# Stage A in seven Strassen products over pairs of token blocks, with the second block's output products moved into the next attention

## The reference, cut to what matters

```
# attention: B=4, H=8, S=768, D=64; chunks of 32 queries see 8 memory keys
# and their own chunk with 16 keys to the left and 8 to the right
for c in range(S // 32):
    scores = scale * q_c @ k_full.T            # 32 x (8 + 16 + 32 + 8) = 32 x 64 keys
    a = softmax(scores)
    out[:, :, c_start:c_end] = a @ v_full
x = out.transpose(0, 2, 1, 3).reshape(3072, 512)

# stage A: d_model 512, d_ff 1536
x = (sigmoid(x @ w_gate) * (x @ w_val)) @ w_out

# stage B: d_model 512, d_ff 2048; P and Q are polynomials in h with given coefficients
h = x @ w_in
g = P(h) / (Q(h) + 1e-6)
return g @ w_out2                              # 3072 x 512, float32
```

## Time and profile before

| | before |
| --- | --- |
| median of three runs | 1231.11 us |
| profiled execution, first to last instruction | 1228.0 us |
| TensorE matmul busy | 1201.9 us (98%) |
| VectorE busy | 733.7 us (60%) |
| ScalarE busy | 644.8 us (53%) |
| GpSimd busy | 127.5 us (10%) |
| DMA moved | 69.45 MB |
| instructions | 21612 |

### The profile page before, as it was taken

The page is one execution under the profiler, slowest core; times in us unless marked ns, Lnnn a source line. Parts: engine busy times, 40 slices in busy tenths (PEclk is TensorE's granted clock), DMA queues, the critical chain, the costliest instruction groups (busy, mean ns, idle before and its releaser), DMA issues.

```text
span 1228.0 us, 21612 instructions
## 1 busy us (share of the span) xinstructions
PE 1201.9 (98%) x8648; PEld 1001.7 (82%) x8648; DVE 733.7 (60%) x1007; ACT 644.8 (53%) x1000; POOL 127.5 (10%) x102
## 2 busy tenths in 40 slices
PE   7999999999999999999999999999999999999998
PEld 6999988878887887888888888788888888888886
DVE  4653322232223223222344599999999999999997
ACT  4654433233223332322333677777777777777775
POOL 0000000000000000000000022222222222222221
PEclk9999999999999999999999999999999999999999
DMA  5751211211211212110322300100200100100000
GB/s 190 242 182 51 99 62 44 72 51 44 87 44 39 84 44 79 45 44 1 120 95 86 112 1 1 51 18 0 68 0 0 68 0 0 68 0 0 35 1 35
DMA packets 30600, 69.45 MB, mean 57 GB/s; under 512 B 3392, under 2 KB 3392, under 8 KB 30528
## 3 DMA queue, kind: packets, MB, share of 16 engines
q1 hardware_dynamic: 30528, 68.37, 16.4%
HBM read 55.77 MB, written 12.58 MB: 56 GB/s over the span
## 4 chain that ended last, share of the span: by engine, by line
PE 51%; DVE 26%; ACT 15%; issue 3%; DMA 3%; SPq 0%; DVEq 0%; POOL 0%; ACTq 0%
DVE unit L586 12%; PE ps_h L629 11%; PE ps_h L630 10%; PE ps_h L634 10%; DVE unit L582 6%; DVE unit L579 5%; ACT unit L429 5%; PE ps_y L736 5%; PE ps_y L737 5%; PE ps_y L740 5%; ACT unit L427 4%; ACT hid L434 3%; DMA wraw<-wa_l 2%; PE ps_h L682 1%; PE ps_h L658 1%
## 5 line engine op out<-in xcount | busy, mean ns | idle before, releaser
L629 PE MATMUL ps_h<-x_split,weights 128*128 128x512 f32 (+1 forms) x1056 | 392.1, 377 | 6.3 <-issue 2.4
L630 PE MATMUL ps_h<-x_split,weights 128*128 128x512 f32 (+1 forms) x1056 | 386.0, 371 | 0.0
L634 PE MATMUL ps_h<-x_split,weights 128*128 128x512 f32 (+1 forms) x1056 | 262.7, 371 | 0.1
L302 POOL TENSOR_TENSOR unit<-unit 128x512 f32<-128x512 f32 x96 | 126.8, 1321 | 1087.2 <-ACT unit L417 1087.2
L629 PEld LDWEIGHTS ps_h<-x_split,weights 128*128 128x128 f32 x1056 | 199.4, 189 | 44.5 <-issue 7.4
L522 DVE TENSOR_TENSOR gated<-ps_h,gated 128x512 f32<-128x512 f32 (+1 forms) x84 | 51.7, 615 | 303.6 <-PE ps_h L634 296.8
L630 PEld LDWEIGHTS ps_h<-x_split,weights 128*128 128x128 f32 x1056 | 199.8, 189 | 32.4
L634 PEld LDWEIGHTS ps_h<-x_split,weights 128*128 128x128 f32 x1056 | 189.1, 189 | 34.6 <-DVE x_split L477 0.6
L586 DVE SCALAR_TENSOR_TENSOR unit<-unit,coefs 128x512 f32<-128x512 f32 x96 | 165.8, 1727 | 3.4
L361 ACT ACTIVATE hid<-gated 128x512 fp32r<-128x512 f32 (+1 forms) x84 | 47.9, 571 | 197.6 <-DVE gated L522 197.6
L355 ACT ACTIVATE gated<-ps_h 128x512 f32<-128x512 f32 (+1 forms) x84 | 45.0, 535 | 166.3 <-PE ps_h L634 166.2
(11 more groups left out here) (84 smaller groups left out, 1482.3 us busy)
## 6 DMA issues: line engine op xcount, KB each, us to landing
unit<-v_l SPq DMA_DIRECT2D x24, 520.0 KB, 5.1
unit<-k_l SPq DMA_DIRECT2D x24, 512.0 KB, 4.3
wraw<-wa_l SPq DMA_DIRECT2D x36, 256.0 KB, 3.4
wraw<-wb_l SPq DMA_DIRECT2D x32, 256.0 KB, 2.7
unit<-q_l SPq DMA_DIRECT2D x24, 256.0 KB, 2.9
y_dram<-stage SPq DMA_DIRECT2D x24, 256.0 KB, 2.3
x_stage<-y_dram SPq DMA_DIRECT2D x6, 1024.0 KB, 5.7
out<-stage SPq DMA_DIRECT2D x24, 256.0 KB, 2.2
```

The lines of the kernel that those rows point to most:

```text
L302: nc.gpsimd.tensor_tensor(quad[s], quad[s], habs[s], ALU.mult).then_inc(q2_done, 1)
L629: nc.tensor.matmul(dst, lhs(c, 0), rhs_hi(c), start=(c == 0), stop=False)
L630: nc.tensor.matmul(dst, lhs(c, 1), rhs_hi(c), start=False, stop=False)
L634: last = nc.tensor.matmul(dst, lhs(c, 0), rhs_lo(c), start=False, stop=(c == KT - 1))
```

## The change

Stage A now takes two token blocks (1024 tokens, a "super-block" `s`, three in all) and two hidden tiles at a time. The 2 x 2 grid of (token block, hidden tile), with the contraction halved as well, is one Strassen-Winograd product with seven products in place of eight: a `chain` of seven products of six matmuls each, one chain for the gate and one for the value. The four results are put together from partial sums that share PSUM banks: ScalarE takes a snapshot of a bank between two products, and VectorE adds it to another bank. The sums of weights that the method needs are made by GpSimd, the sums of x by VectorE. The weights of stage A no longer stay in SBUF: gate and value weights are loaded, summed and split for every chain (36 chains), and the output weights for every output piece (72 pieces of 256 KB) through rings of two and three buffers.

The output products of the first token block of a pair run between the chains. Those of the second block run between the steps of the next eight attention units, which are taken two at a time. The first eight units run before any product. After the last chain the second block's pieces run alone, while stage B's weights come in through a ring of four buffers; stage B's block 0 is taken out of the hardware loop. All of stage A is written out, without a hardware loop.

The diff, cut to its core (`quad_a` is the pair of chains as ScalarE and VectorE see it):

```diff
+M1, M2, M6, M5, M7, M3, M4 = range(PROD)
+STEPS = [(0, "P", True), (1, "Q", True), (4, "P", False), (3, "R", True), (5, "P", False), (6, "R", False),
+         (2, "P", False)]
...
+        B_BEHIND = [range(0, 4)] + [range(3 * i + 1, 3 * i + 4) for i in range(1, 9)] + [range(28, 30), range(30, 31),
+                                                                                        range(31, 32)]
...
SP queue
+            def load_qk(g):
+                b = g % 2
+                wait(sp, scores_done, g - 1)
...
+            def load_v(g):
+                b = g % 2
+                wait(sp, pv_done, g - 1)
...
+            def load_oraw(n):
+                wait(sp, wo_lo, n - ORING + 1)
...
+                for p in range(UNITS // 2):
+                    if p < 3:
+                        for g in range(UNITS * (s + 1) + 2 * p + 2, UNITS * (s + 1) + 2 * p + 4):
+                            load_qk(g)
+                    load_oraw(piece_of(s, 1, 2 * p))
+                    if p == 0:
+                        store_a(2 * s, 0)
+                        store_a(2 * s, 1)
+                    if p < 3:
+                        for g in range(UNITS * (s + 1) + 2 * p + 2, UNITS * (s + 1) + 2 * p + 4):
+                            load_v(g)
+                    load_oraw(piece_of(s, 1, 2 * p + 1))
+                    if p == 0:
+                        store_a(2 * s, 2)
+                        store_a(2 * s, 3)
...
+            for f in range(TA):
+                for n in B_BEHIND[f]:
+                    load_braw(n)
+                if f == 0:
+                    for m in range(4):
+                        store_a(NT - 2, m)
+                if f + 2 < TA:
+                    load_oraw(piece_of(NS - 1, 1, f + 2))
...
GpSimd
+            def weight_sums(c):
...
+                nc.gpsimd.tensor_tensor(s1, a21, a22, ALU.add).then_inc(s_made, 1)
+                pool.wait_ge(s_made, 4 * c + 1)
+                nc.gpsimd.tensor_tensor(s2, s1, a11, ALU.subtract).then_inc(s_made, 1)
+                nc.gpsimd.tensor_tensor(s3, a11, a21, ALU.subtract).then_inc(s_made, 1)
+                pool.wait_ge(s_made, 4 * c + 2)
+                nc.gpsimd.tensor_tensor(s4, a12, s2, ALU.subtract).then_inc(s_made, 1)
...
ScalarE
+            def quad_a(u):
...
+                split_w(cg + 2, 0)
+                split_w(cg + 2, 1)
+                snapshot(cv, 0)
+                split_w(cg + 2, 2)
+                snapshot(cv, 1)
+                split_hid(u, 0)
+                snapshot(cv, 2)
+                split_w(cg + 2, 3)
+                split_hid(u, 1)
+                split_hid(u, 2)
+                split_hid(u, 3)
...
+            for o in (T2, T1, T3, B22, T4):
+                for c in range(2):
+                    split_x(0, o, c)
...
+                for p in range(1, UNITS // 2):
+                    g = UNITS * (s + 1) + 2 * p
+                    exp_scores(g)
+                    exp_scores(g + 1)
...
+                    split_wout(piece_of(s, 1, 2 * p))
+                    copy_turned(g)
+                    copy_turned(g + 1)
+                    split_wout(piece_of(s, 1, 2 * p + 1))
...
+                    stage_x(g)
+                    stage_x(g + 1)
...
VectorE
+                split_w(cg + 2, 3)
+                split_hid(u, 1)
+                chain_sum(cv, 2)
+                value(u, 2)
+                value(u, 3)
+                split_hid(u, 2)
+                split_hid(u, 3)
...
TensorE
+            def chain(c):
+                u, kind = divmod(c, 2)
+                s, i = divmod(u, NQ)
+                pe.wait_ge(w_lo, 4 * (c + 1))
+                for m, (w, name, first) in enumerate(STEPS):
...
+                    elif m == M6:
+                        pe.wait_ge(snap_done, 3 * c + 1)
...
+            for s in range(NS):
+                for i in range(NQ):
+                    u = NQ * s + i
+                    chain(2 * u)
+                    if i:
+                        out_piece(s, 0, 2 * i - 2)
+                        out_piece(s, 0, 2 * i - 1)
+                    chain(2 * u + 1)
...
+                for p in range(1, UNITS // 2):
+                    g = UNITS * (s + 1) + 2 * p
+                    scores(g)
+                    scores(g + 1)
+                    out_piece(s, 1, 2 * p - 2)
+                    turn(g, True)
+                    turn(g + 1, True)
+                    out_piece(s, 1, 2 * p - 1, (0,))
+                    weigh_values(g)
+                    weigh_values(g + 1)
+                    out_piece(s, 1, 2 * p - 1, (1, 2))
+                    turn(g, False)
+                    turn(g + 1, False)
+                for f in range(UNITS - 2, TA):
+                    out_piece(s, 1, f)
+            out_piece(NS - 1, 0, TA - 2)
+            out_piece(NS - 1, 0, TA - 1)
+            for f in range(TA):
+                out_piece(NS - 1, 1, f)
```

More of the change, by code:

```diff
@@ L43 @@
 ONE_EPS = 1.0 + 1e-6
[L44 to L62 removed]
+NS = NT // 2
@@ new lines, in turn @@
+            def turn(g, first):
+                b = g % 2
+                if first:
+                    pe.wait_ge(exped, g + 1)
+                else:
+                    pe.wait_ge(norm_done, g + 1)
+                for h in range(HP):
+                    last = nc.tensor.transpose(ps_att[b][:, 0, P * h:P * (h + 1)],
+                                               probs[b][:, h].rearrange("p s k -> p (s k)"), ident[:])
+                last.then_inc(turned_done if first else xturn_done, 1)
```

1133 lines of the change are left out of this document (708 added, 425 removed).

## The result

The changed kernel took 1309.42 us (median of four runs, 1305.85 to 1313.72), beside 1231.03 us before (1230.37 to 1231.57). The ratio is 1.064, with a 95% interval of 1.0618 to 1.0663: it is 78 us slower. I had forecast 1278 us, slower, with a range of 1215 to 1301. The direction was right, the loss is 1.7 times as large as I said, and the time lies outside the range.

The account below looks back on a forecast made before the run. TensorE's matmuls, filling 98% of the span, were taken as the bound. Start 60.5, chains 441, attention 182, end 57 and stage B 534.7 sum to 1275; with 3.1 added, 1278 us, range 1215 to 1301.

Parts of the forecast that it names:

- TensorE's savings: Work removed from TensorE: 216 chain matmuls 49.0 us, block 0's halved matmuls 5.8, loop turns about 7; near 62 us.
- The start: Time before the first chain, eight attention units with no products under them: 60.5 us, including 1.5 for the clock; bounds 50 and 66.
- My sum of a pair: Prologue path of two attention units, from scores through softmax and values to staging and hand-overs: 10.5 us.
- The chains: Three super-blocks' products and output pieces: 424.4 us of work plus waits, 441 us; bounds 424 and 460.
- The snapshot's stop: In the chains, ScalarE's next snapshot stands behind two splits: 0.8 us for each of 15 pairs, 12 us.
- The attention: Two phases between super-blocks: each 61.3 us work, 29 waits and 1 for the clock; 182 us in all.
- 1 us for the clock after idles over 3 us (as in part 1): Allowance per attention phase for TensorE's clock falling to half after idling, as the start had taken 1.5 us.
- The end: Stage A's last pieces, bound by the turn of stage B's four weight buffers: 57 us; bounds 43 and 62.
- B: Rival: attention loads are hidden, pieces land in 2.7 us, each phase waits 12 us, not 29; 1244 us, chance 0.18.
- C: Rival: faster, TensorE stays the bound in attention and at the end, weights always arriving in time; 1224 us, chance 0.2.
- D: Rival: GpSimd's sums hold VectorE at the critical splits in the chains, 23 us more; 1301 us, chance 0.1.
- a clock that stays low over whole phases: One of three stated signs that the forecast is wrong: TensorE's granted clock staying low through entire phases.

Follow-up runs that it names:

- before_unrolled: The kernel before the change with TensorE's hardware loop over blocks 1 to 4 written out; 1227.85 us, ratio 0.997 to before.
- warm5: The changed kernel with 5 warm-up matmuls in place of 10 at each prologue place, 15 in place of 30 before the first chain; 1307.32 us.
- snap_sum_first: The changed kernel with ScalarE's next snapshot and VectorE's next first sum ahead of the last two hidden-value splits; 1295.77 us.
- snap_first: The changed kernel with ScalarE taking the next chain's first snapshot before the last two hidden-value splits; 1308.61 us.
- keep_clock: The changed kernel with spare 128-column matmuls filling part of TensorE's waits in the attention phases; 1295.93 us.
- ring8: The changed kernel with eight buffers in place of four for stage B's weights; 1297.85 us in a single run.
- thin_units: The changed kernel with q, k and v of units 8 to 23 loaded in 64 columns only (output not the reference's); 1281.38 us, single run.
- out_first: The changed kernel with output-weight loads issued before the next units' q, k and v in SP's queue during attention; 1272.0 us.
- pool_narrow: The changed kernel with GpSimd's four weight sums on 16 of 256 columns (output not the reference's); 1308.99 us, single run.

## Why the prediction was right in kind and short in size

- **TensorE's savings** (62 us). The 648 matmuls of stage A went as counted, 55 us. The loop's turns were priced too high: before_unrolled gains 3.6 us where I had about 7. Stage B is right: 535.7 against 534.7 us.
- **The start** (60.5). Pairs of units came 12.7 and 13.1 us apart (scores at 21.03, 33.69 and 46.84; 10.5 predicted). My sum of a pair has no term for the warm-up matmuls, three times ten of them, and ten cost 2.4 us; warm5 shows that they are part of it (its second pair takes 10.9 us). Behind the staging the sum was 0.9 us too long. The clock loss that I named for TensorE's idling did not occur: the windows from 40 to 72 us all stand at 1.00. It appears once there are fewer warm-ups, in warm5. The first chain starts 3.6 us later than I said; with its own stop, which the table counts to the chains, the start is 5 us short.
- **The chains** (441). The snapshot's stop is where I put it and costs what I said: 0.69 us idle, nearly 0.8 us of a pair by snap_sum_first, against 0.8. snap_first shows that ScalarE was not alone: VectorE's splits are late for the same reason. But even without the stop a pair takes 24.9 us, and its 108 steps of 0.2267 make 24.5, so pairs are 25.65 us apart against 25.3: 5 us over 15 pairs. The first pair of a super-block has the one stop that I had, 1.6 us predicted, 1.22, 1.58 and 1.58 us measured. GpSimd costs nothing, as priced. 8.2 us short with the first chain's stop, some 7 without it.
- **The attention** (182). This is the step that failed, in the words "1 us for the clock after idles over 3 us (as in part 1)". Idles of the first phase: 2.46, 0.95, 8.44, 2.78, 4.06, 2.99, 1.59, 0.81, 2.51 and 1.41, 28.0 us in all, against 29 predicted. In the second phase they are 32.1 us. So the sum of the waits was nearly right, partly by luck: the first piece came later behind the v loads (6.6 us against 4.3), 4 us a phase are waits for instructions inside groups of small matmuls, which no step of mine had, and the last waits were shorter. What I missed is the work between the waits: 70.7 and 70.0 us of busy time, where I had 61.3 + 1. That is 16 of the 18.8 us by which the two phases are longer than forecast. keep_clock shows some 7 us a phase of it to be the clock; the small matmuls' own pace can be the rest, and no run separates it. I had taken the clock once a phase, from one idle of 3 us in the prologue; the first attention phase has four idles of 2.8 us and more, and the first alone leaves a whole piece at half the clock (1.9 us more).
- **The end** (57). Right: 57.1 us, with the ring as its bound, which ring8 shows in a single run.
- **The rivals.** B and C asked for landings within 3 us of the issue. In the change a piece lands after 4.8 us there (median), so they did not come. Their condition was not the one that decides: thin_units has the landings (2.8 us) and phases of 86 and 88 us, out_first has the short phases (78 and 81 us) with landings of 4.3. What counts is how early a piece is asked for. D is excluded by pool_narrow.

The condition "over 3 us" in the step that failed does not hold either. This is a window of the change:

```profile
217.00:220.00 3.00, 2.84 (x130) 2.60 (x131) 3.00 (x5) 2.89 (x4) 0.00 (x0) 0.50 0.16 33
```

It stands at half the clock behind an idle of 2.45 us. In out_first the same work, from 218.6 to 221.6 us, stands at 1.00 behind an idle of 2.46 us. So whether the clock falls is not settled by the length of the one idle before. One of my signs of being wrong, a clock that stays low over whole phases, came half true: 0.83 and 0.85 in the mean.

The range was too narrow above, because each long idle was paid once in it. An idle and the clock after it belong together: where the waits are uncertain, so is the clock.

## What to carry over

Where small work on TensorE waits on other engines several times in a row, price the longer waits (here those of some 2.5 us and more) twice, once as idle time and once as the work behind them, which may run at the 0.43 us step. Before removing matmuls, ask what other work lay under them: here 49 us of products went, and six units of attention lost their cover. In a queue that a hand-written order serves, a load that an engine awaits before its next hand-over belongs ahead of the large loads that are wanted later; two lines were worth 37 us.

## What the runs showed of the hardware that I had not expected

- TensorE stops, mostly for 1.5 to 3 us, at fixed places of its program inside runs of 128 small matmuls, with no semaphore as releaser. Each stop ends 1.2 to 1.6 us after a 16 KB packet of the instruction queue q8 has ended. Splitting the runs into 64 leaves the places where they are and shrinks the stops a little (8.6 to 6.8 us in the attention).
- A stop of 0.69 us on TensorE costs more than itself: pairs are 0.8 us shorter without it. The first matmul behind one takes longer to its successor (0.34 and not 0.23 us at 68.03 in the change).
- GpSimd's float32 sum over 256 columns takes 0.74 us alone and 0.94 to 1.17 us beside VectorE's splits; VectorE's split of a hidden value takes 0.69 us alone and up to 1.23 beside it.
- The DMA engines hold some 400 GB/s over 20 us when enough is in flight (ring8).
- A turn of TensorE's hardware loop costs 0.6 to 1.2 us of idle time.
